# The decay of a linear-attention state: eight ScalarE copies in place of one VectorE multiply

## The reference

```python
for t in range(S):
    kt, vt, rt, wt = (k[:, :, t], v[:, :, t], r[:, :, t], w[:, :, t])
    cur = np.einsum('bhd,bhe->bhde', u[None] * kt, vt)
    y[:, :, t] = np.einsum('bhd,bhde->bhe', rt, state + cur)
    state = wt[:, :, :, None] * state + np.einsum('bhd,bhe->bhde', kt, vt)
...
h = x @ w_in                                  # layer 2, d_ff 2048
g = h * np.clip(h + 3.0, 0.0, 6.0) / 6.0
x = g @ w_out
...
silu(xn @ w_gate) * (xn @ w_val) @ w_out      # layer 3 on RMS-normed x, d_ff 1536
```

## Time and profile before

| | us |
|---|---|
| median of 3 runs | 935.53 (934.98 to 935.71) |
| the profiled execution | 935.66 |
| its span | 933.9 |
| PE busy in it | 921.6 |
| DVE, ACT, POOL busy | 521.3, 361.7, 291.9 |

### The profile page before, as it was taken

One profiled execution on the slowest core, in us unless ns is written; L12 is line 12 of the kernel. 1 busy time (PEld: TensorE's weight loads), 2 busy tenths in 40 slices (PEclk: granted clock), 3 DMA queues, 4 the chain that ended last, 5 costly groups with the idle time before them and its releaser, 6 DMA issues.

```text
span 933.9 us, 17547 instructions
## 1 busy us (share of the span) xinstructions
PE 921.6 (99%) x7064; PEld 772.9 (83%) x7064; DVE 521.3 (56%) x752; ACT 361.7 (39%) x786; POOL 291.9 (31%) x244
## 2 busy tenths in 40 slices
PE   7999999999999999999999999999999999999998
PEld 7899988888888888888888888888888888888886
DVE  6888976566666666315774553553463373363332
ACT  4557454354444445336463123223223223223212
POOL 4789544454454444324351011011011001101000
PEclk9999999999999999999999999999999999999999
DMA  9874442233223231014221010010000001000000
GB/s 255 237 208 129 109 131 60 63 105 86 75 61 107 69 83 51 22 39 135 86 83 45 0 35 34 1 34 34 0 34 35 1 19 50 0 1 34 1 1 34
DMA packets 33008, 60.40 MB, mean 65 GB/s; under 512 B 6112, under 2 KB 19936, under 8 KB 32928
## 3 DMA queue, kind: packets, MB, share of 16 engines
q1 hardware_dynamic: 27104, 50.82, 18.7%
q10 hardware_dynamic: 5824, 8.47, 3.1%
HBM read 47.66 MB, written 9.44 MB: 61 GB/s over the span
## 4 chain that ended last, share of the span: by engine, by line
PE 93%; DVE 4%; issue 1%; DMA 1%; ACT 1%; SPq 1%; DVEq 0%; ACTq 0%
PE acc L1079 34%; PE bank L1050 11%; PE bank L1052 11%; PE bank L1051 11%; PE pair L1050 5%; PE pair L1051 5%; PE pair L1052 5%; DVE ki L731 1%; PE acc L1113 1%; PE pair L1132 1%; PE pair L1189 1%; PE pair L1161 1%; DVE cum L719 1%; PE bank L1068 1%; PE bank L1153 1%
## 5 line engine op out<-in xcount | busy, mean ns | idle before, releaser
L1079 PE MATMUL acc<-gs,w_dn 128*128 128x512 f32 (+1 forms) x1512 | 357.0, 382 | 1.2 <-issue 1.2
L1079 PEld LDWEIGHTS acc<-gs,w_dn 128*128 128x128 f32 x1512 | 272.9, 188 | 55.1 <-issue 1.3
L945 POOL TENSOR_TENSOR gs<-act_g,gs 128x512 fp32r<-128x512 f32 (+1 forms) x96 | 122.1, 1272 | 208.3 <-ACT gs L550 208.2
L1050 PE MATMUL bank<-xs,w_up 128*128 128x512 f32 (+1 forms) x459 | 171.9, 374 | 1.4 <-DVE state L762 1.2
L1052 PE MATMUL bank<-xs,w_up 128*128 128x512 f32 (+1 forms) x459 | 169.1, 368 | 0.0
L1051 PE MATMUL bank<-xs,w_up 128*128 128x512 f32 (+1 forms) x459 | 169.0, 368 | 0.0
L801 DVE SCALAR_TENSOR_TENSOR act_g<-act_u,bank 128x512 f32<-128x512 f32 (+1 forms) x112 | 67.5, 603 | 139.8 <-ACT act_u L542 139.8
L869 DVE TENSOR_TENSOR act_u<-act_u,bank 128x512 f32<-128x512 f32 x72 | 49.5, 688 | 146.8 <-ACT act_u L612 146.8
L542 ACT ACTIVATE act_u<-bank,half 128x512 f32<-128x512 f32 (+1 forms) x112 | 70.0, 625 | 150.8 <-PE bank L1052 139.9
L616 ACT ACTIVATE gs<-act_g 128x512 fp32r<-128x512 f32 x72 | 45.5, 632 | 155.9 <-DVE act_g L875 155.9
L1050 PEld LDWEIGHTS bank<-xs,w_up 128*128 128x128 f32 x459 | 86.4, 188 | 18.0 <-DVE state L762 1.6
(11 more groups left out here) (121 smaller groups left out, 1121.6 us busy)
## 6 DMA issues: line engine op xcount, KB each, us to landing
rkn<-in_rkN SPq DMA_DIRECT2D x22, 384.0 KB, 4.1
rkt<-in_rkT SPq DMA_DIRECT2D x44, 192.0 KB, 3.6
val<-in_valN SPq DMA_DIRECT2D x22, 256.0 KB, 3.0
x<-x_dram SPq DMA_DIRECT2D x6, 768.0 KB, 4.2
dec<-in_decT SPq DMA_DIRECT2D x46, 97.5 KB, 2.3
x_dram<-xo SPq DMA_DIRECT2D x5, 768.0 KB, 4.1
out<-xo SPq DMA_DIRECT2D x5, 768.0 KB, 3.3
raw_dn<-in_w_out SPq DMA_DIRECT2D x14, 192.0 KB, 4.8
```

The lines of the kernel that those rows point to most:

```text
L945: pool.tensor_tensor(gs[:, f % GRING, 1, tok], act_g[:, f % 2, tok], gs[:, f % GRING, 0, tok].bitcast(F32), ALU.subtract).then_inc(s_glo, 1)
L1050: pe.matmul(dst, w_hi, x_hi, start=first, stop=False)
L1079: last = pe.matmul(ps_o[m][:, tok], w[:, wp, m * P:(m + 1) * P], gs[:, f % GRING, xp, tok], start=f == 0 and a == 0, stop=f == nf - 1 and ...
```

## The change

`scale_state` moves from VectorE to ScalarE. On VectorE it was one TENSOR_TENSOR of 112 x 384, with `last` broadcast along the columns. On ScalarE it is eight ACTIVATE copies of 112 x 48, in place, each with its factor per partition. The place is the same phase, PREP: on ScalarE that is behind `g_hi` of the step and ahead of `up_gate` of the next one (in pass 0, where there is no `g_hi`, behind `up_gate` and ahead of the weight splits). ScalarE waits for the two updates of the state and for its own `keep_last`.

```diff
+            def scale_state(g):
+
+                act.wait_ge(s_state, STATE_INCS * g + 2)
+                act.wait_ge(s_last, g + 1)
+                for p in range(PAIRS):
+                    for b in range(PB):
+                        part = state[0:DP, g % SETS, p, b, :]
+                        n = p * PB + b
+                        done = act.activation(part, part, ACT.Copy, scale=last[0:DP, g % LASTS, n:n + 1])
+                done.then_inc(s_state, 1)
+
...
+                if phase == PREP and has_state(g) and not is_first(g):
+                    scale_state(g)
...
-            def scale_state(g):
-
-                dve.wait_ge(s_state, STATE_INCS * g + 2)
-                old = state[0:DP, g % SETS, :, :, :].rearrange("p a b d -> p (a b) d")
-                dve.tensor_tensor(old, old, last[0:DP, g % LASTS, :].unsqueeze(2).broadcast_to([DP, PAIRS * PB, D]),
-                                  ALU.mult).then_inc(s_state, 1)
...
-                    if has_state(g) and not is_first(g):
-                        scale_state(g)
```

## The result

The change makes the kernel slower by a little. The ratio of the changed kernel to the one before is 1.0024, with a 95% interval of 1.0013 to 1.0034, from 20 runs of each: medians 936.37 (934.99 to 938.32) and 933.69 us (930.81 to 938.22). On 933.7 us the ratio is +2.2 us, +1.2 to +3.2. The forecast was +1.2 and a median of 936.7. The three runs of before that stood beside the prediction (median 935.53) lie near the upper end of the 20.

What follows compares the result with a forecast made beforehand. PE was taken to bound the kernel (busy 921.6 of 933.9 us), with VectorE setting its time only at two MEETs in pass 1. 2.05 - 0.45 - 0.4 = +1.2 us on 935.53 gave 936.7, range 934.8 to 938.3.

Steps and rivals of the forecast that it cites:

- The bound and the place: PE bounds the kernel; only pass 1 can change, while pass 0 and passes 2 to 5 hide copies and missing multiply.
- The copies: ScalarE, each group: eight copies 0.22 us apart hold it 1.8 us, priced from the 128 x 64 `att` row.
- Group 4: Pass 1, steps 2 to 6: late scan waits out GpSimd's run, ending at 83.8; PE loses 2.05 us.
- Group 5: Pass 1: scan and `rd` nearly coincide, so the 0.9 us wait goes or stays; booked as -0.45 us.
- Group 6: Pass 1, steps 10 to 14: scan meets an idle GpSimd, the 0.3 us wait goes; gain 0.4 us.
- The sum: Whole kernel: 2.05 - 0.45 - 0.4 = +1.2 us on a median of 935.53, so 936.7.
- slower by over 0.2%: Whole kernel: time above 937.4 us, given a chance of 0.18.
- B: Rival, pass 1: scan enters behind one instruction, sum -0.4 us, 935.1, up to 935.9; chance 0.33 together with nothing happening.
- C: Rival, pass 1: ScalarE becomes the late engine, a second block in a later group; +2.9 us, 938.4; chance 0.14.
- D: Rival, pass 1: VectorE's relief removes `update_state` waits and the longer DMA wait; 1.5 us faster, 934.0; chance 0.05.

Runs made afterwards that it cites:

- e3: Changed kernel, but ScalarE scales the state only in groups 4 to 7 (pass 1) and VectorE in the other 16; ratio to before 1.0025.
- e4: Changed kernel, but VectorE scales the state in groups 4 to 7 (pass 1) and ScalarE in the other 16; ratio to before 1.0001.
- e2: The changed kernel, unedited, profiled and timed a second time; ratio to before 1.0019.
- e10: Kernel before, VectorE still scaling, plus eight ScalarE copies into unused memory in PREP of groups 4, 5 and 6; ratio to before 1.0012.
- e11: Changed kernel with each group's copies moved to the next group's MEET, in step 1 of a pass behind the accumulator copies (`xo`); ratio to before 0.9981.
- e7: Changed kernel with the scaling of the state left out on either engine, ScalarE only raising the semaphore; ratio to before 0.9991.
- e1: The kernel before, unedited, profiled and timed a second time; ratio to before 1.0007.
- e12: Changed kernel with copies in the next group's MEET, behind the accumulator copies, and GpSimd waiting behind `rd` for the scan; ratio to before 0.9976.

## Why the prediction was right

**The bound and the place.** Right. PE's work and everything outside pass 1 stayed equal (807.79 and 807.75 us behind it), and e3 and e4 show that passes 0 and 2 to 5 hide both the copies and the missing multiply.

**The copies.** 1.8 us were forecast for eight, 1.90 measured as their length and 1.80 from the first copy's start to the next `up_gate` (78.48 to 80.28). By the row of 128 x 64, then, a good price.

**Group 4.** Forecast: the scan in its turn at 80.3, behind POOL's `rd`, `w_dn` and `gs`, ending at 83.8. At its scores PE stood 0.83 us later in this trace than in the first (83.96 against 83.13), from the start of the program and the wait named issue. Less that, the scan came at 80.28 and ended at 83.42. The start was right to 0.02 us. The end was 0.4 us early, because GpSimd, without the multiply beside it, reached `rd` at 79.45 by the same reckoning and not at 79.8. PE came to step 6 by 88.85 - 86.30 - 0.83 = 1.72 us late; 2.05 were forecast, or 2.1 by the prediction's own rows, in which PE goes on 0.94 us after `hidden` has started (99.16 to 100.10) and not 0.88. One step was missing: PE meets VectorE's lateness twice, first at the sums, which wait for `hidden` of the step before, and then ahead of step 6.

**Group 5, the step that failed.** I booked -0.45, halfway between 0 and -0.9, on the ground that the scan and `rd` would come at nearly the same time. The scan came 0.40 us into `rd` (94.14 against 93.74) and took 2.91 us, and in e2 the same. The waits are 0.22 + 0.88 = 1.10, against 0.89: +0.2 in place of -0.45.

**Group 6.** Forecast: scan at an idle GpSimd, the wait gone, 0.4 us gained. The scan took its least time, 1.23 us, the wait is gone, and by how much PE is behind the first trace of before fell by 0.40 us between the keys of step 11 and those of step 15 (1.54 to 1.14).

**The sum.** Between the first two traces pass 1 grew by 57.66 - 56.80 = 0.9 us, the spans by 1.1. The terms gave +1.2, and that these are close is in part luck. The wait named issue is 0.73 us shorter in the second of the two traces; without these waits pass 1 grew by 1.6, and the terms as measured give 1.72 + 0.2 - 0.4 = 1.5. The medians grew by 2.2, and what lies behind that is the base: I took the trace's 0.89 and 0.31 us for properties of the kernel before, and let the change earn 0.4 + 0.45 by removing them. In the second trace of before they are absent. Against an execution like that one the change earns nothing: its four waits of 0.45 + 0.88 + 0.22 + 0.88 = 2.4 us count in full, and with the longer rows around them pass 1 is 56.96 - 53.70 = 3.3 us longer. The +2.2 us of the medians lie between 0.9 and 3.3, as they would if the executions of before were of both kinds; how often each kind comes is not shown. The median of 936.7 was met within 0.4 us by luck: three runs of before had given a base 1.8 us above that of twenty, and the change was taken 1.0 us too small. The chance of "slower by over 0.2%" should have been the greater one.

**The rivals.** B, that the scan enters behind one instruction, was not the case here (three in group 4, two in group 5), but it is what e10 shows. The rule named beside it from SBUF — State Buffer of the Trainium skill, section "Who interferes with whom", that the shared pair of ports goes to one engine for a whole instruction, agrees with the rows of both: the scan's row ends 1.10 us after `gs` has ended, nearly its whole 1.23, so it had done next to nothing before; and `rd`, where a scan got in ahead of it, takes 2.12 us in place of 1.19. C came about in part, measured against the second trace of before: group 5 was also blocked. D needed the copies to fit into 0.77 us; e11 shows that its gain was to be had, with the copies elsewhere.

## What to carry to other kernels

An engine with idle time in the mean may have none where the work is put: count the idle time ahead of the next instruction that another engine waits for (0.77 us here, against copies of 1.8), and put work whose reader is far off behind the instructions with near readers, `up_gate` and `xo` among them. A scan that started 0.63 us later ended 2.3 us later, since it had lost its place in front of another engine's run on a shared port; a wait that makes the other engine give way bought it back. Before booking a gain from a wait that a trace shows, look at a second trace of the same kernel for it.

## What the runs showed of the hardware

**Who gets the port next.** The timelines of VectorE and GpSimd in pass 1 of all kernels, e7 left out, give an order that I had not expected. A scan that comes during `gs` and finds `rd` next gets in ahead of `rd`, in all 15 cases; it takes 1.38 to 1.45 us in 13 of them, and 1.23 us in the two in which `gs` had at most 0.12 us to go. A scan that comes 0.3 us or more into `rd`, with GpSimd's next instruction ready, lets at least that one pass in 19 of 21 cases; the two that enter at once came 0.44 us into it, in pass 1's last group. A scan that comes 0.09 us behind the start of `rd` enters behind it, in both cases. What decides between these is open.

**Waits named issue.** A wait of PE of 0.2 us or more that no engine ends comes at three matmuls of the program and nowhere else up to pass 2, in some executions and not in others of one kernel: at 17 to 21 us (1.05 to 3.24 us long, in 13 of the 14 traces), in `across` of group 4 (0.24 to 0.53, in 9) and in a `down` of step 6 (0.21 to 1.25, in 5). The packets of the DMA queue that the profile calls instruction go with them. They have 16 KB each, and at each of the 27 waits PE goes on 1.2 to 1.7 us after such a packet has ended; where it does not wait at these places, the last one had ended at least 1.3 us before. In the first trace of before the packet runs from 86.96 to 88.04 us and PE goes on at 89.39, after 1.25 us; in the second it runs from 84.45 to 85.78, and PE passes the place at 87.36 without a wait. It looks as if PE waits there for its own program. No run moves a packet, so this is a pairing too, and why it comes late is open.

**The start of the program.** Between 20 and 25 us the first trace of before has a mean granted clock of 0.66, between the levels of 2.4 and 1.2 GHz, behind the wait of 2.75 us that ends at 20.46. The second trace of after has no such wait, and 1.00:

```profile
20.00:25.00 5.00, 4.54 (x69) 4.29 (x69) 1.65 (x4) 2.60 (x6) 3.05 (x4) 0.66 0.99 247
20.00:25.00 5.00, 4.65 (x33) 4.02 (x32) 4.17 (x7) 2.47 (x6) 4.92 (x5) 1.00 1.04 271
```

That the wait brings the clock down is not shown: e4 has one of 1.96 us there and stays at 1.00. But the two go with the time. The transposes at step 7 of pass 0 begin at 38.31 us in the second trace of after, where the other traces have 39.67 to 42.28, and of the 105 executions of before beside e1 to e12 the nine with a mean clock of 1.00 took 931.4 us on the mean, the other 96 took 934.4. The 4 us at the start, and the 3.1 us in pass 1 between the two traces of before (56.80 and 53.70), are together of the size of the 7 us between the fastest and the slowest run of that kernel; a difference of 2 us between two single traces says nothing here.
